# Which chunks of a gated convolution are rounded and which get their middle tap by DMA, on an attention + FFT mixing + MLP kernel (one core)

## What is computed

```python
# 1. linear attention, 4 batches x 4 heads x 1088 tokens x 32
phi(x) = outer(S1 x, S2 x)                      # 64 features
x = (phi(q) @ (phi(k)^T v)) / (phi(q) . sum phi(k))   -> x: 4 x 1088 x 128
# 2. mixing block
u  = x + real(fft(fft(x, tokens), channels))
un = (u - mean(u)) / sqrt(var(u) + 1e-6)
x  = u + relu(un @ w_ch1) @ w_ch2               # 128 -> 512 -> 128
# 3. gated convolution block
h  = relu(x @ w_in)                             # 128 -> 1024
conv = w[0] h[s-1] + w[1] h[s] + w[2] h[s+1]    # along tokens, per channel
out = (h * sigmoid(conv)) @ w_out               # 1024 -> 128
```

## Time and profile before

| | us |
|---|---|
| median of 3 runs | 251.67 (251.54 to 251.69) |
| the profiled execution, its own time | 252.02 |
| its span in the profile | 250.2 |
| PE busy | 242.9 |
| DVE busy | 215.4 |
| ACT busy | 170.8 |
| POOL busy | 53.3 |

### The profile page before, as it was taken

The page is one execution under the profiler, slowest core; times in us unless marked ns, Lnnn a source line. Parts: engine busy times, 40 slices in busy tenths (PEclk is TensorE's granted clock), DMA queues, the critical chain, the costliest instruction groups (busy, mean ns, idle before and its releaser), DMA issues.

```text
span 250.2 us, 4440 instructions
## 1 busy us (share of the span) xinstructions
PE 242.9 (97%) x1558; PEld 215.1 (86%) x1558; DVE 215.4 (86%) x408; ACT 170.8 (68%) x334; POOL 53.3 (21%) x123
## 2 busy tenths in 40 slices
PE   8999999999999999998989999999999999999995
PEld 6999999999989998997978877998879879797753
DVE  0747888899998697899899999988969999989992
ACT  2452634332576566667799898999958989997852
POOL 0000000000624530665501332031421211321100
PEclk9999999999999999999999999999999999999999
DMA  6968830210000020000004799387988446997602
GB/s 194 392 243 320 344 101 3 62 40 0 3 0 0 4 84 1 3 3 3 0 0 89 186 261 217 141 165 195 262 206 158 135 134 181 280 196 157 170 3 89
DMA packets 9094, 31.41 MB, mean 126 GB/s; under 512 B 1264, under 2 KB 2032, under 8 KB 9072
## 3 DMA queue, kind: packets, MB, share of 16 engines
q0 software_dynamic: 4752, 18.35, 30.8%
q1 hardware_dynamic: 4176, 12.74, 14.1%
q10 hardware_dynamic: 144, 0.03, 0.1%
HBM read 10.54 MB, written 2.23 MB: 51 GB/s over the span
## 4 chain that ended last, share of the span: by engine, by line
PE 41%; DVE 11%; ACT 2%; issue 1%; ACTq 0%
PE ps L707 10%; PE ps L613 9%; PE ps L615 9%; PE ps L614 9%; PE ps L656 4%; DVE attic L1196 4%; DVE attic L1203 3%; DVE attic L1181 2%; DVE late_lo L1114 1%; PE ps L647 1%; ACT folded_room L900 1%; ACT arena L829 1%; DVE x2lo L1127 0%; ACT attic L915 0%; DVE wout_lo L1213 0%
## 5 line engine op out<-in xcount | busy, mean ns | idle before, releaser
L915 ACT ACTIVATE attic<-attic,base 128x1088 f32<-128x1088 f32 x32 | 37.9, 1204 | 4.6 <-DVE attic L1196 4.5
L707 PE MATMUL ps<-attic,wout 128*128 128x364 f32 (+1 forms) x120 | 39.1, 469 | 0.1
L613 PE MATMUL ps<-x2hi,wlo 128*128 128x364 f32 x96 | 37.2, 388 | 0.8 <-ACT folded_room L900 0.7
L707 PEld LDWEIGHTS ps<-attic,wout 128*128 128x128 f32 x120 | 22.5, 189 | 13.2 <-issue 2.1
L615 PE MATMUL ps<-x2hi,whi 128*128 128x364 f32 x96 | 31.6, 329 | 0.0
L614 PE MATMUL ps<-x2lo,whi 128*128 128x364 f32 x96 | 31.5, 328 | 0.0
L613 PEld LDWEIGHTS ps<-x2hi,wlo 128*128 128x128 f32 x96 | 18.1, 188 | 4.9 <-ACT folded_room L900 1.7
L900 ACT ACTIVATE x_room<-ps 128x364 f32<-128x364 f32 x42 | 18.3, 479 | 4.0 <-PE ps L615 3.7
L458 POOL TENSOR_SCALAR arena<-arena 109x4 f32<-109x4 f32 x10 | 2.0, 197 | 88.4 <-DVE arena L1099 88.3
L1196 DVE SCALAR_TENSOR_TENSOR attic<-x_room,ratio,attic 128x1088 f32<-128x1088 f32 x14 | 18.7, 1348 | 1.7 <-DMA attic<-x_room 1.6
L614 PEld LDWEIGHTS ps<-x2lo,whi 128*128 128x128 f32 x96 | 18.1, 188 | 2.4 <-issue 1.1
(11 more groups left out here) (130 smaller groups left out, 621.6 us busy)
## 6 DMA issues: line engine op xcount, KB each, us to landing
gate_hi<-attic POOLq DMA_DIRECT2D x12, 544.0 KB, 3.5
attic<-folded_room POOLq DMA_DIRECT2D x9, 544.0 KB, 5.0
attic<-x_room POOLq DMA_DIRECT2D x8, 544.0 KB, 5.3
attic<-v_d SPq DMA_DIRECT2D x4, 594.0 KB, 3.8
attic<-qT_d SPq DMA_DIRECT2D x3, 545.0 KB, 7.0
attic<-kT_d SPq DMA_DIRECT2D x3, 544.5 KB, 6.1
attic<-arena POOLq DMA_DIRECT2D x3, 544.0 KB, 5.3
out_d<-arena SPq DMA_DIRECT2D x3, 544.0 KB, 4.7
```

The lines of the kernel that those rows point to most:

```text
L613: pe.matmul(out, lo, rhi, start=first, stop=False)
L707: pe.matmul(ps[:, OUT_BANK + t, 0:z - a], wout[:, c, :], gate(i)[:, a:z], start=(c == 0), stop=(c == C2 - 1)).then_inc(wout_done, 1)
L915: act.activation(gate(i), gate(i), ACT.Sigmoid, scale=base[:, i % C2:i % C2 + 1]).then_inc(gate_ready, 1)
```

## The change

Six constants and one place in VectorE's slot:

- CAST: chunks 3 and 8 are added, 17 is taken out (12 -> 13 chunks, 2 to 8 without a gap).
- ADDED: 10 is added, 8 and 27 are taken out (20 -> 19): chunks 8 and 27 become plain.
- SCALED: 17 and 28 are taken out: their scaled copy is ScalarE's.
- LAGS: lag 7 now also at i = 28, lag 6 from i = 29 (before: 6 at 28 and 29, 5 from 30). So hidden(28) is followed by the projection of 21 alone (before 21, 22), hidden(29) by 22, 23 (before 23), hidden(30) by 24 (before 24, 25), hidden(31) by 25 to 31 (before 26 to 31).
- In slot 19 VectorE does `normed_low(6)`, the low half of the seventh unit, ahead of `mixed_rows(9)` instead of behind it.

```diff
-ADDED = (4, 6, 7, 8, 9, 11, 12, 13, 15, 16, 17, 18, 20, 22, 24, 25, 26, 27, 28, 30)
-CAST = (2, 4, 5, 6, 7, 11, 12, 13, 16, 17, 20, 21)
+ADDED = (4, 6, 7, 9, 10, 11, 12, 13, 15, 16, 17, 18, 20, 22, 24, 25, 26, 28, 30)
+CAST = (2, 3, 4, 5, 6, 7, 8, 11, 12, 13, 16, 20, 21)
 CASTS = 3
-SCALED = (11, 17, 28)
+SCALED = (11,)
...
-LAGS = ((-1, 7), (28, 6), (30, 5))
+LAGS = ((-1, 7), (29, 6))
...
                 if n < NC1 and has_low(n):
                     hidden_low(n)
+                if n in TURNS_AT and n == 19:
+                    normed_low(TURNS_AT[n])
                 if n in MIXED_AT:
                     mixed_rows(MIXED_AT[n])
...
-                if n in TURNS_AT:
+                if n in TURNS_AT and not n == 19:
                     normed_low(TURNS_AT[n])
```

## The result

The changed kernel takes **253.82 us** (median of seven runs), the kernel before 251.69 on the same chip: a ratio of 1.0068 (95% interval 1.0052 to 1.0084), about 1.7 us slower by the ratio (the two medians differ by 2.1 us). Forecast were 251.1 us and a range that ended at 252.3.

A forecast was written before the change was run, and what follows sets the result against it. VectorE was taken to bound until 142.9 us, TensorE's stream after 145.6. Roundings -0.33, chunk 12 wait +0.1, slot 19 -0.1 and lags -0.27 gave -0.6 us: 251.1 us from 251.67, range 250.5 to 252.3.

The forecast's parts named there:

- Roundings -0.33: TensorE's gapless stream: chunks 3 and 8 rounded, 17 plain, shortening it by 0.33 us.
- Lags -0.27: Tail: TensorE's wait before projection 30 goes, -0.27 us, with bounds of 0 and -0.27.
- The taps as totals: Taps moved between routes add work on VectorE and ScalarE, neither the limit after 146 us: no cost as totals.
- I put 0.1 us on the sum: Hidden product of chunk 12: margin 0.2 us if no DMA is late; 0.1 us allowed for the rounding of 3.
- The list of starts: VectorE's predicted starts from right tap 4 at 141.50 through low 2 at 142.76 to product 6 at 155.65.
- my bound: Chunk 12: if the rounding of 3 takes 5.0 us, VectorE waits 1.4 and TensorE has a hole of 1.2 us.
- It is late by more than 0.7 us: Rounding of 8, issued about 162.1, low half due about 165.5; later by over 0.7 us delays chunk 15's hidden product.
- The early low halves stall TensorE: Rival: wait at chunk 12's hidden product, up to 1.2 us, if the rounding of 3 exceeds 3.8 us; chance 0.25.
- chunk 15 late as well, up to 252.9: Worse form of the early-low-halves rival: chunk 15's hidden product also waits, time up to 252.9 us; rival's chance 0.25.
- Slot 19: Low half ahead of mixed rows: TensorE starts 1.0 us earlier near 114 us, but VectorE sets the pace; -0.1 us.
- The danger that I named there: Slot 19: a left tap at 119.03 starts before POOL's step of 119.08, holds it, and gives back all the gain.
- What I had said would show it: Signs: right tap 4 within 0.3 us of 141.5; low 3 within 0.2 of VectorE free; first wait at chunk 12.

The follow-up runs named there:

- the roundings alone: The kernel before with only the change's CAST (which chunks are rounded): 251.54 us, ratio 0.9982.
- the lags alone: The kernel before with only the change's LAGS: 251.46 us, ratio 0.9980.
- changed again: The changed kernel run again with no edit, against the kernel before: 253.36 us, ratio 1.0058.
- the first profile: First profiled execution of the changed kernel, no further edit; that kernel measured 253.82 us, ratio 1.0068 against the kernel before.
- two of them together: The kernel before with the change's CAST and LAGS, its own taps and slot 19 order: 251.30 us, ratio 0.9968.

## Why the prediction was wrong

**What bounds it, and the gains: right.** TensorE's stream sets the time after 146 us, and its gains came nearly as costed. Roundings -0.33: the profile of the roundings alone ends 0.24 earlier; rounding 8 gives 0.29. Lags -0.27: 0.28 in the lags alone, 0.29 in the changed kernel. The taps as totals cost nothing: 0.9998.

**"I put 0.1 us on the sum" for chunk 12: the mechanism was right, the size was off.** Product 6 was predicted for 155.65 and started at 156.21. The list of starts had the low half of 2 at 142.76. It started at 143.07, since it still waits for its own rounding, as before (143.14). That wait stands in the trace of before, and the list drops it without a reason. It did not go: the rounding took 4.86 us with nothing behind it for 2.4 us. That is 0.31 of the 0.56; 0.11 more come at the low half of 3, whose rounding landed at 144.35, and 0.13 at the right tap of 8. The prediction read the 5.0 us of this rounding as the price of the addition 1.2 us behind it; the counts (2.92 us for the fifteenth in before, 2.93 in changed again) and the run with nothing behind it say that it is not. The rounding of 3, on which my bound hung, was harmless: 3.7 us, inside my 3.0 to 3.7. The holes measured 0.44 (with that at 13) and, in the first profile, 0.74, of a bound of 1.2.

**"It is late by more than 0.7 us": this is the failed step.** The rounding of chunk 8 got a sentence and a condition, and no term. I had it issued at 162.1, the low half due at 165.5, and 0.7 us of tolerance. Measured on the chain:

- projection 5 ends at 162.68: +0.58, of which 0.44 are the holes at 12 and 13,
- from there to the start of the DMA: +0.56, which I had left out,
- the rounding takes 4.60 us, not 3.4: +1.20. Its fifteenth count came after 3.27 us, so the 3.4 held for all but the last.

Together 2.34 us; less the tolerance of 0.7 and TensorE's own lateness of 0.44 this is 1.20, and the hole is 1.16. Rows 7 had the size: two of twelve roundings took 4.8 and 5.0 us, and I allowed the 5.0 for chunk 3 but not for chunk 8. With 4.8 instead of 3.4, and the 0.5 us of issue, the condition would have read 1.9 against 0.7 and given a hole of 1.2 us as a term: 251.1 + 1.2 = 252.3, slower than before even with chunk 12 as forecast. What the rows did not have is a rule by neighbours. In the trace of before six roundings started with an addition under way; they took 3.68, 3.79, 3.26, 3.67, 4.85 and 4.57 us, and as such I had named the 4.8 alone.

**The rival had the right case, not its cause.** "The early low halves stall TensorE", with "chunk 15 late as well, up to 252.9", is what happened, at a chance of 0.25, and the range left out just that double hole. The time went beyond even the 252.9. And the rival's condition, a rounding of 3 of over 3.8 us, did not come true (3.70): the first hole came by the rounding of 2, so that the rival named chunk 12 rightly was in part luck.

**Slot 19.** I took -0.1 and the runs can't tell it from nothing. TensorE does get its transposes 1.06 us earlier, and then waits for the low half of the token unit, which VectorE makes when it did before. The changed kernel, all engines, against the earlier trace rows:

```profile
113.76 0.59 PE L626 MATMUL ps<-ident,arena 109*128 109x109 f32 x4
...
115.65 0.66 DVE L1127 TENSOR_TENSOR x2lo<-ps,x2hi 128x218 fp32r<-128x218 f32 x2
...
116.82 0.41 PE L613 MATMUL ps<-x2hi,wlo 128*128 128x364 f32 x1 [0.62 <-DVE x2lo L1127]
...
122.57 0.86 DVE L1106 TENSOR_SCALAR arena<-x_room,arena 109x128 f32<-109x128 f32 x3 [0.65 <-POOL arena L472]
```

The danger that I named there, a tap that starts just ahead of a GpSimd step and holds it, shows in the kernel with chunks 8 and 10 on their old routes, by 0.05 us:

```profile
119.22 1.35 DVE L1183 SCALAR_TENSOR_TENSOR attic<-x_room,ratio 128x1088 f32<-128x1088 f32 x1
119.27 1.35 POOL L464 TENSOR_TENSOR arena<-arena 109x4 f32<-109x4 f32 x1
...
122.90 0.60 DVE L1106 TENSOR_SCALAR arena<-x_room,arena 109x128 f32<-109x128 f32 x2 [0.95 <-POOL arena L472]
```

L464 takes 1.35 us instead of 0.20, and the last rows come at 122.90 where they came at 122.57. Counted from hidden 0 it costs 0.15 us at hidden 10 in this execution, and the same in that of the changed kernel without the rounding of 8. But in both, hidden 0 had come 0.15 us early against the matmuls of 111 us, so the step only gave back what the new order had gained, as the prediction feared. The first profile of the changed kernel gained 0.14 there and kept it; the other six executions with the new order neither gained nor lost. The rule of the Trainium skill that the prediction named (SBUF — State Buffer, "Who interferes with whom") agrees with these two records.

**What I had said would show it.** The first hidden product with a wait was indeed chunk 12's, released by the ReLU; VectorE's wait for the rounding of 3 was at most 0.1 us, and right tap 4 stayed at 141.53. All three hold, and the kernel is slower: I had set no sign for the rounding of 2 or for chunk 15.

## What to carry to other kernels

An instruction that waits for a DMA costs what stands behind it on its engine: give each such wait a due time and a price of its own, from the slowest of its kind in the trace, and put it behind, not ahead of, whatever frees a buffer for the bounding engine. A wait that stands in the trace of before stays in the forecast until something is shown to remove it. Parts of a change that use up the same slack are added up against it. Run the parts in pairs as well as alone: here two of them together gave 0.3%, and all of them lost 0.6%.

## What the runs showed of the hardware

**The same DMA takes 2.9 to 6.2 us.** A rounding is 544 KB from SBUF to SBUF, always the same. In the changed kernel between 138 and 164 us it landed after 2.9 us (issued at 149.44 and 157.79, each with one addition right behind), 3.7 (140.65 and 147.16), 4.60 (163.24, with two additions behind), 4.86 (138.19, with no other rounding or addition in flight and none behind it for 2.4 us) and 6.2 (158.99, 0.67 us behind an addition). Two things are mixed here. In the 6.2 us all sixteen counts are late (the fifteenth after 5.94), which goes with the addition ahead of it; in the 4.60 and 4.86 only the last is, which goes with an instruction packet. The additions of 544 KB took 5.3 us in the median. From the Trainium skill (DMA: Bandwidth & Descriptors, "Anatomy of one DMA — SWDGE (gpsimd) path"), a fixed 2.0 us and 436 GB/s, one would estimate 3.3 us for it; the traces lie about it where neither thing happens (2.9 to 3.7 us), and at up to nearly twice as much where one does.

**Every execution has a shift of its own.** In all but the first profile of the changed kernel, hidden 0 lay between -0.69 and +0.50 us of before's, and what stands behind it moves with it. There the first product of the attention's features starts between 6.9 and 8.1 us, but the two go together only loosely (with the roundings alone 0.21 us earlier than before, and hidden 0 0.41 later), so where the shift comes from is not shown. It is as large as the effects sought here, so two profiled executions are compared only after it is subtracted.
